# Expert stage of a one-core delta-rule and mixture-of-experts kernel: bulk transfers issued by ScalarE, copies of w1 left to the sync engine, sorted rows stored tile by tile

## What is computed

```python
# attention, per batch and head, over t
y[t] = q[t] @ state
state = state + beta[t] * outer(k_n[t], v[t] - k_n[t] @ state)
# experts: E = 8, F = 1024
e_idx = argmax(x @ w_gate + modality_bias[modality_id]);  gate_w = its softmax probability
out[mask_e] = gate_w * (relu(x[mask_e] @ w1[e]) @ w2[e])
# second layer: F2 = 768
h = maximum(maximum(x @ m2_w1, x @ m2_w2), x @ m2_w3);  result = h @ m2_out
```

## Time and profile before

| | us |
|---|---|
| median of 3 runs | 1092.8 (1092.8 to 1100.61) |
| the profiled execution | 1095.86 |
| its span | 1094.1 |
| mean granted clock of TensorE | 0.964 |
| TensorE busy in the span | 918.4 |
| ScalarE busy in the span | 480.7 |

### The profile page before, as it was taken

One profiled execution on the slowest core, in us unless ns is written; L12 is line 12 of the kernel. 1 busy time (PEld: TensorE's weight loads), 2 busy tenths in 40 slices (PEclk: granted clock), 3 DMA queues, 4 the chain that ended last, 5 costly groups with the idle time before them and its releaser, 6 DMA issues.

```text
span 1094.1 us, 29171 instructions
## 1 busy us (share of the span) xinstructions
PE 918.4 (84%) x10418; PEld 679.9 (62%) x10418; DVE 623.9 (57%) x1484; ACT 480.7 (44%) x1076; POOL 308.5 (28%) x810
## 2 busy tenths in 40 slices
PE   3258989888798888238998998997799999999998
PEld 3147878777797778226776776765554454545444
DVE  5337778767777767624884865943763324243322
ACT  3124656556465545624853736633542323323221
POOL 4646456767857553520000000001430000000000
PEclk9999889989989999659999999998999999999999
DMA  6366665655434441079639669479840000000000
GB/s 154 73 167 175 165 156 118 146 102 113 101 83 94 91 99 31 16 254 356 221 146 316 252 235 329 187 275 325 274 146 8 22 29 1 29 0 29 7 22 29
DMA packets 223333, 147.07 MB, mean 134 GB/s; under 512 B 162240, under 2 KB 200128, under 8 KB 223200
## 3 DMA queue, kind: packets, MB, share of 16 engines
q1 hardware_dynamic: 170208, 126.42, 37.2%
q10 hardware_dynamic: 49920, 9.44, 4.6%
q0 software_dynamic: 3072, 9.44, 2.7%
HBM read 69.63 MB, written 26.87 MB: 88 GB/s over the span
## 4 chain that ended last, share of the span: by engine, by line
PE 47%; POOL 15%; SPq 13%; issue 9%; DMA 8%; DVE 4%; ACT 2%; another core or an unknown queue 1%; DVEq 0%; POOLq 0%; ACTq 0%
PE psum L1617 19%; PE psum L1636 6%; PE psum L1566 5%; PE psum L1553 5%; POOL arena L637 4%; POOL arena L634 3%; SPq L554 3%; DMA arena<-arena 2%; SPq L529 2%; SPq L510 2%; DMA arena<-blocks 2%; SPq L558 2%; DMA arena<-in_moe_w_dram 1%; POOL arena L665 1%; PE psum L1470 1%
## 5 line engine op out<-in xcount | busy, mean ns | idle before, releaser
L1617 PE MATMUL psum<-arena 128*128 128x512 f16 x972 | 212.4, 379 | 0.3 <-issue 0.3
L1553 PE MATMUL psum<-arena 128*128 128x128 f16 x2232 | 148.8, 222 | 23.7 <-DMA arena<-arena 18.2
L1617 PEld LDWEIGHTS psum<-arena 128*128 128x128 f16 x972 | 95.0, 98 | 112.4 <-issue 0.7
L1553 PEld LDWEIGHTS psum<-arena 128*128 128x128 f16 x2232 | 135.8, 99 | 41.4 <-DMA arena<-arena 20.6
L1566 PE MATMUL psum<-arena 128*128 x744 | 144.1, 330 | 20.2 <-DVE arena L1211 9.1
L804 POOL DMA_INDIRECT arena<-y_sorted,arena x24 | 23.6, 982 | 319.2 <-DMA y_sorted<-arena 288.1
L1314 DVE SCALAR_TENSOR_TENSOR arena<-psum,arena 128x512 f32<-128x512 f32 x36 | 27.0, 751 | 146.5 <-PE psum L1617 146.5
L1566 PEld LDWEIGHTS psum<-arena 128*128 128x128 f16 x744 | 71.4, 97 | 59.6 <-issue 33.6
L971 ACT ACTIVATE arena<-psum 128x256 f16<-128x256 f32 x124 | 46.9, 378 | 95.8 <-PE psum L1553 90.0
L1211 DVE SCALAR_TENSOR_TENSOR arena<-psum,arena 128x256 f16<-128x256 f32 x124 | 52.1, 420 | 59.5 <-ACT arena L971 57.3
L1140 DVE SCALAR_TENSOR_TENSOR arena<-arena 128x384 f16<-128x384 f32 x128 | 73.1, 613 | 13.6 <-ACT arena L830 8.3
(11 more groups left out here) (198 smaller groups left out, 1807.4 us busy)
## 6 DMA issues: line engine op xcount, KB each, us to landing
arena<-arena SPq DMA_DIRECT2D x124, 384.0 KB
arena<-in_moe_w_dram SPq DMA_DIRECT2D x73, 384.0 KB, 4.8
arena<-inverses SPq DMA_DIRECT2D x24, 512.0 KB, 5.8
x_sorted<-arena SPq DMA_DIRECT2D x7, 768.0 KB, 6.0
arena<-in_k_dram SPq DMA_DIRECT2D x24, 192.0 KB, 3.7
arena<-in_v_dram ACTq DMA_DIRECT2D x24, 192.0 KB, 3.7
arena<-in_q_dram ACTq DMA_DIRECT2D x24, 192.0 KB, 4.5
out_dram<-arena SPq DMA_DIRECT2D x24, 192.0 KB, 1.9
```

The costliest lines, as they stand in the source:

```text
L1553: last = nc.tensor.matmul(psum[:, n % 2, fc * P:fc * P + P], w1[:, at:at + P], xT16[:, s, y, kc * P:kc * P + P], start=(i == 0), stop=(i = ...
L1617: last = nc.tensor.matmul(psum[:, 2 + 3 * (f % 2) + m, :], up_weight(w, m, kc, f), x16[:, par, kc, x, :], start=(i == 0), stop=(i == len(t ...
```

## The change

The loads of the experts' and the second layer's weights, the last three loads of sorted rows and the stores to y_sorted move from the sync engine to ScalarE, inside its loop over tiles, behind the ReLU (and, in pass 0, the turned rows) and ahead of square sums and splits: weight i at tile i + 1, store of tile s - 2 at tile s. Each store now covers one tile, with a count per part. The sync engine's loop holds only copies of w1. Square sums, total and splits of the second layer's weights come one tile later than before; those of the experts' weights (`weighed_in`, `split_in`) stay.

```diff
         LG = DM
         CUM = 2 * P
         SX = [0, 1, 3, 6, 11, 18, 24, NSLOT]
+        FIRST = 4
         block = ctx.enter_context(nc.Block())
-        AHEAD = 3
         HALVES = (slice(0, PC // 2), slice(PC // 2, PC))
         def weighed_in(s):
...
         def m2_weighed_in(s):
-            return [s - 3] if 3 <= s < NM + 3 else []
+            return [s - 4] if 4 <= s < NM + 4 else []
         def m2_split_in(s):
-            return [s - 17] if 17 <= s < NM + 17 else []
-        M2_SUMMED, M2_SCALED = 15, 16
+            return [s - 18] if 18 <= s < NM + 18 else []
+        def part_of(s):
+            return sum(1 for z in SY[1:-1] if s >= z)
+        M2_SUMMED, M2_SCALED = 16, 17
         ROWS_SUMMED, ROWS_SCALED, TURNED = (24, 25), 26, 27
         SPLIT = NT - 4
...
         def columns_after(f, last):
             return [] if last else {1: [0, 1], 3: [2]}.get(f, [])
+        def expert_weights(queue, qq, i):
+            e, f0 = i // 2, qq * FQ
+            if i % 2 == 0:
+                queue.dma_start(raw(qq, i).rearrange("p (c f) -> p c f", c=KC),
+                                w1[e, :, f0:f0 + FQ].rearrange("(c p) f -> p c f", p=P)).then_inc(w_in[i // 4], 16)
+            else:
+                queue.dma_start(raw(qq, i).rearrange("p (c n) -> p c n", c=FC),
+                                w2[e, f0:f0 + FQ, :].rearrange("(c p) n -> p c n", p=P)).then_inc(w_in[i // 4], 16)
+        def load_columns(queue, i):
+            a, z = SX[i], SX[i + 1]
+            queue.dma_start(acc[:, a:z, :], x_sorted[a * P:z * P, :].rearrange("(s p) d -> p s d", p=P)).then_inc(xs_in[i], 16)
         def groups_in_order(e, group):
...
             sp.dma_start(cst16[:, :], c16).then_inc(cst_in, 16)
             sp.dma_start(cst32[:, :], c32).then_inc(cst_in, 16)
             sp.dma_start(braw[0:B * H, :], beta.rearrange("b h s -> (b h) s")).then_inc(beta_in, 16)
-            def expert_weights(qq, i):
...
             def step(what, t):
                 if what == "k":
...
                                  inverses[pair % 2, :, t % 2].rearrange("p h x c -> p (h x c)")).then_inc(inv_in[t % 4], 16)
                 if what == "w":
                     if 4 <= t < 4 + 2 * E:
-                        expert_weights(0, t - 4)
+                        expert_weights(sp, 0, t - 4)
                     if 6 <= t < 14:
                         a, z = NSLOT * (t - 6) // 8, NSLOT * (t - 5) // 8
                         sp.dma_start(x_sorted[a * P:z * P, :].rearrange("(s p) d -> p s d", p=P),
                                      zrow.unsqueeze(1).to_broadcast([P, z - a, DM])).then_inc(zero_in, 16)
-            def load_columns(i):
-                a, z = SX[i], SX[i + 1]
-                sp.dma_start(acc[:, a:z, :], x_sorted[a * P:z * P, :].rearrange("(s p) d -> p s d", p=P)).then_inc(xs_in[i], 16)
             def copy_w1(n):
...
             sp.wait_ge(scat_in, 16 * NT)
             sp.wait_ge(s_ok, NT)
-            for i in range(4):
-                load_columns(i)
+            for i in range(FIRST):
+                load_columns(sp, i)
             sp.wait_ge(eid_ok, 1)
             sp.wait_ge(gate_ok, 3)
-            for n in range(AHEAD):
+            for n in range(NQ * NSLOT):
                 copy_w1(n)
-            def m2_weights(i):
...
-            def store_sorted(i):
-                a, z = SY[i], SY[i + 1]
-                sp.wait_ge(acc_ok, NSLOT * (NQ - 1) + z)
-                sp.dma_start(y_sorted[a * P:z * P, :].rearrange("(s p) d -> p s d", p=P), acc[:, a:z, :]).then_inc(ysort_in[i], 16)
-            for n in range(NQ * NSLOT):
-                qq, s = n // NSLOT, n % NSLOT
-                if n + 4 < len(SX) - 1:
-                    load_columns(n + 4)
-                if s < NP and qq < NQ - 1:
-                    if s == 0 and qq > 0:
-                        sp.wait_ge(ym_mm, NSLOT * qq)
-                    expert_weights(qq + 1, s)
-                if s < NM and qq == NQ - 1:
-                    if s == 0:
-                        sp.wait_ge(ym_mm, NSLOT * (NQ - 1))
-                    m2_weights(s)
-                if qq == NQ - 1 and s - 1 in SY[1:]:
-                    store_sorted(SY.index(s - 1) - 1)
-                if n + AHEAD < NQ * NSLOT:
-                    copy_w1(n + AHEAD)
-            store_sorted(NC - 1)
             with sp.Fori(0, NC) as c:
                 for b in range(B):
...
                 c = t // B
                 if t % B == 0:
                     pool.wait_ge(h_mm, NSLOT * (NQ - 1) + B * (c + 1))
-                    pool.wait_ge(ysort_in[c], 16)
+                    pool.wait_ge(ysort_in[c], 16 * (SY[c + 1] - SY[c]))
                 nc.gpsimd.indirect_dma_start(x2[:, t, :], None, y_sorted[0:SY[c + 1] * P, :],
                                              bass.IndirectOffsetOnAxis(ap=pos[:, t:t + 1], axis=0)).then_inc(gath_in[min(c, 2)], 16)
...
                 need(act, o_mm, c * B)
                 nc.scalar.activation(h16[:, f, 0], h2[:, f % 2, :], ACT.Copy).then_inc(hhi_ok, 1)
+            def m2_weights(i):
+                if i < 3 * KC:
+                    act.dma_start(m2_raw(i), (m2_w1, m2_w2, m2_w3)[i // KC][i % KC * P:(i % KC + 1) * P, :]).then_inc(w_in[i // 3], 16)
+                else:
+                    f = 2 * (i - 3 * KC)
+                    act.dma_start(m2_raw(i).rearrange("p (c n) -> p c n", c=2),
+                                 m2_out[f * P:(f + 2) * P, :].rearrange("(c p) n -> p c n", p=P)).then_inc(w_in[i // 3], 16)
+            def store_sorted(s):
+                act.wait_ge(acc_ok, NSLOT * (NQ - 1) + s + 1)
+                act.dma_start(y_sorted[s * P:s * P + P, :], acc[:, s, :]).then_inc(ysort_in[part_of(s)], 16)
+            act.wait_ge(scat_in, 16 * NT)
+            for i in range(FIRST, len(SX) - 1):
+                load_columns(act, i)
             columns(0)
             columns(1)
             for qq in range(NQ):
...
                     nc.scalar.activation(hT[:, n % 2, 0, :], psum[:, n % 2, 0:FQ], ACT.Relu).then_inc(hh_ok, 1)
                     if qq == 0 and s + 2 < NSLOT:
                         columns(s + 2)
+                    if s == 1 and qq > 0:
+                        act.wait_ge(ym_mm, NSLOT * qq)
+                    if qq < NQ - 1 and 1 <= s <= NP:
+                        expert_weights(act, qq + 1, s - 1)
+                    if qq == NQ - 1 and 1 <= s <= NM:
+                        m2_weights(s - 1)
+                    if qq == NQ - 1 and s >= 2:
+                        store_sorted(s - 2)
                     if qq < NQ - 1:
                         for i in weighed_in(s):
                             weigh(qq + 1, i)
...
                                 square_row(0, 0, B // 2 * ROWS_SUMMED.index(s) + b)
                         if TURNED < s <= TURNED + KC:
                             x_high(0, 0, s - TURNED - 1)
+            for s in (NSLOT - 2, NSLOT - 1):
+                store_sorted(s)
             def group(c, par, last):
                 for f in range(F2C):
```

More of the change, by code:

```diff
@@ L473, in _ @@
             sp.dma_start(braw[0:B * H, :], beta.rearrange("b h s -> (b h) s")).then_inc(beta_in, 16)
-            def expert_weights(qq, i):
-                e, f0 = i // 2, qq * FQ
-                if i % 2 == 0:
-                    sp.dma_start(raw(qq, i).rearrange("p (c f) -> p c f", c=KC),
-                                 w1[e, :, f0:f0 + FQ].rearrange("(c p) f -> p c f", p=P)).then_inc(w_in[i // 4], 16)
-                else:
-                    sp.dma_start(raw(qq, i).rearrange("p (c n) -> p c n", c=FC),
-                                 w2[e, f0:f0 + FQ, :].rearrange("(c p) n -> p c n", p=P)).then_inc(w_in[i // 4], 16)
             def step(what, t):
@@ L563, in _ @@
             sp.wait_ge(s_ok, NT)
-            for i in range(4):
-                load_columns(i)
+            for i in range(FIRST):
+                load_columns(sp, i)
             sp.wait_ge(eid_ok, 1)
             sp.wait_ge(gate_ok, 3)
-            for n in range(AHEAD):
+            for n in range(NQ * NSLOT):
                 copy_w1(n)
-            def m2_weights(i):
-                if i < 3 * KC:
-                    sp.dma_start(m2_raw(i), (m2_w1, m2_w2, m2_w3)[i // KC][i % KC * P:(i % KC + 1) * P, :]).then_inc(w_in[i // 3], 16)
-                else:
-                    f = 2 * (i - 3 * KC)
-                    sp.dma_start(m2_raw(i).rearrange("p (c n) -> p c n", c=2),
-                                 m2_out[f * P:(f + 2) * P, :].rearrange("(c p) n -> p c n", p=P)).then_inc(w_in[i // 3], 16)
-            def store_sorted(i):
-                a, z = SY[i], SY[i + 1]
-                sp.wait_ge(acc_ok, NSLOT * (NQ - 1) + z)
-                sp.dma_start(y_sorted[a * P:z * P, :].rearrange("(s p) d -> p s d", p=P), acc[:, a:z, :]).then_inc(ysort_in[i], 16)
-            for n in range(NQ * NSLOT):
-                qq, s = n // NSLOT, n % NSLOT
-                if n + 4 < len(SX) - 1:
-                    load_columns(n + 4)
```

(13 more changed lines are left out.)

## The result

The changed kernel takes 1144.55 us in the median (1137.13 to 1152.45, 4 runs), the kernel before 1095.15 in the runs beside it: a ratio of 1.0445, 95% interval 1.0358 to 1.0531. Slower was forecast, at 1112 and at most 1135. The sum behind that was +19.5 us; the loss is 49 us, outside the range. The profiled execution took 1141.96 us, 46.1 more than the one of before.

What follows compares the result with a forecast made beforehand. It took the sync engine's queue of copies and loads to bound the expert stage's loading tiles. Passes 1 to 3 +10, +6.8, +6.3, last pass -8.6, clock +5 gave +19.5 us: 1112 us, range 1080 to 1135.

Steps and rivals of the forecast that it cites:

- the last pass: Last pass of the expert stage: weight loads and tile-by-tile stores on ScalarE, -8.6 us, ends -18 and 0.
- part 4: TensorE's clock falls in half of the 12 waits, 0.8 us each: +5 us, ends 0 and +17.
- part 2: Passes 1 to 3: ScalarE waits for loads only just issued, +10, +6.8 and +6.3 us.
- the landing of 4.4 us: Passes 1 to 3: time from issue of an awaited weight load until its data are in, 4.4 us.
- 5.2 us for the three tiles behind a wait: Passes 1 to 3: after a wait, one tile at ScalarE's 1.75 us, two at TensorE's 1.98, less TensorE's lead: 5.2.
- The tiles behind them stay as they are: Passes 2 and 3: tiles after tile 17 keep their time, 0 us.
- Part 1: Sync engine without the loads: a loading tile's bound falls from about 2.5 to 1.98 us, if DMA keeps up.
- The start: Start of pass 1: sorted rows requested at once share DMA engines with the first copy, +4 us, ends 0 and +8.
- C: Rival, slower: landing 5.6 us (+14) and the clock falls mostly (+8), 1134 us; chance 0.12.
- A: Rival, faster: loads land in 3.1 us on ScalarE's queue, -12 us, 1081 us; chance 0.2.
- B: Rival, no difference: landing near 3.7 us, no clock fall, about 1096 us; chance 0.2.
- D: Rival: copies wait for DMA bandwidth, loading tiles stay at 2.5 us; sum changes by 3 at most; no separate chance.

Runs made afterwards that it cites:

- The short loads: Changed kernel with the expert weight loads of passes 2 to 4 cut to 128 and 192 KB, the rest not loaded: ratio 1.0215.
- The one-tile experiment: Changed kernel with only the square sums of the experts' weights one tile later: ratio 1.0021.
- the mended change: Changed kernel with the experts' square sums two tiles later and totals one tile later, splits kept: ratio 1.008.
- the sync engine's version: Kernel before with experts' square sums two tiles and totals one tile later, all transfers left on the sync engine: ratio 0.9985.

## Why the prediction was wrong

**What held.** The direction, and the main cause: ScalarE's in-order wait for load 4g + 3, 12 times in the first three passes, one right behind each issue, with the next ReLU behind it. The signs named for it came: 12 waits, long times from one ReLU to the next behind tiles 4, 8, 12 and 16 (5.6 to 7.8 us, where 5 to 6.5 were named), the clock at 0.50 behind a wait. Their size was off: waits of 3 to 4 us and about 40 in sum were named, and 4.7 and 56.2 came. The 40 did not fit the prediction's own sum either, which holds 12 waits of 4.3 us, 52. Undoing the distance removed the loss, and creating it elsewhere brought it back. The last stage did not change (the time after the last ReLU, +0.9).

**Where the sum missed.** The trace lost 46.1 us for 19.5, so 26.6 are to be explained. By differences of the ReLU rows, against the prediction's own terms: the times over the twelve waits +7.7; the tiles behind the waits +15.9 (10.7 in the groups of three, 5.2 behind the fourth wait of each pass), less the 5 that part 4 had put aside for the clock; the last pass +7.5; the rest and rounding +0.5. So three steps failed, all of them sizes, and the wait itself is not the largest.

**The first step that failed: the landing of 4.4 us in part 2**, and with it "while TensorE stands no new copies come, so I go a little under". It was taken from the median of all loads, and the median was right even afterwards: 4.2 us for ScalarE's loads on the page. But the load that decides is the last of four, issued when three before it and the copies are still moving. In pass 2 the first four landed after 3.9, 5.3, 5.9 and 6.9 us, each later than the one before. By the prediction ScalarE would have idled 0.28 + 4.4 - 0.38 = 4.3 us; it was 5.3 in the mean of the eight waits of passes 2 and 3 (42.0 us), and 3.6 in pass 1 (14.2), where tiles are longer and ask for less per us. The 0.28 was too long, which hid a part: the issue starts 0.01 us behind the ReLU's start (592.89, 592.90), so the awaited load landed after 5.6 us in the mean of these eight and 4.0 in pass 1. The short loads show that most of this is bytes and not a fixed time. In those tiles a load and a copy, 768 KB per 1.98 us, ask for 397 GB/s; the DMA engines gave 361 and 390 in the stretches from 592 to 596 us. Before, the sync engine's loop of 2.5 us asked for about 315 GB/s, which is near the 325 that the earlier trace rows show.

For pass 2 the sum is off by 8.7 us. The ReLU pairs over the four waits were 7.8, 6.5, 6.1 and 7.4, with 5.5, 5.5, 6.3 and 6.3 forecast: 4.2 of it. In pass 3 this step is worth 3.7, in pass 1 nothing.

**The second step, and the largest: 5.2 us for the three tiles behind a wait, nothing for those behind the fourth, and the clock of part 4.** They took 7.6 and 6.9 us after the waits at tiles 4 and 8, with 5.2 forecast, and 7.8 after tile 12, with 7.4: 4.5 us, the other half. The first such wait left TensorE idle for 3.17 us, not 2.4, and the next 24 matmuls took 4.23 us for 2.32. Over the kernel TensorE is busy 14.7 us more, where +5 was put, with an upper end of 17. The idle time was 3.1 us in the mean of the twelve, not 2.4, and the clock fell behind nine of them, not six; so there were 1.6 us of added busy time for each fall, where part 4 had put a loss of 0.8. "The tiles behind them stay as they are" had no reason behind it: behind the fourth wait, gaps of 3.6 to 4.7 us stood at tile 19, and the tiles from 17 on took, over the three passes, 98.6 us for 93.4. With the waits taken out and the splits kept they took 94.2. The one-tile experiment shows the other side, where at 2 us of wait both the delay and the added busy time are gone.

**The third step: the last pass**, -8.6 forecast, -1.1 in the two traces. The gap of the big store went as said (tile 15: 7.7 to 1.4 us), but gaps of 3.9 to 5.1 us stood at tiles 16, 19, 23, 27 and 30. With one and the same code for this pass it took 83.7, 76.9, 76.9, 87.7, 77.9 and 85.1 us in six profiled kernels; so the term can't be read from one trace. The runs with the stores alone put it at -3 us of the kernel (0.9971), and with later sums at nothing (1.0002). What makes these late gaps is open; the trace names "remote" for the one at tile 16.

**Part 1** was right as to the sync engine and wrong as to its worth. Its 2.5 us loop was the path, and a ceiling of the DMA engines lay just behind it, as the 0.95 share of the earlier trace rows said; 39 us had been reckoned for the 17 tiles by bytes, but 43 to 45 came. The rule of the Trainium skill cited there, that a second issuer saves only issue time, is borne out: 281 to 295 GB/s came from two queues and 305 to 310 from one. The mended change against the sync engine's version shows that here even this issue time buys nothing. The start was +6.7 us, forecast +4 with an end of +8; that the table shows +3.8 beside +4 is luck, since the attention stage ended earlier in that trace.

**The rivals.** C gave 1134, the nearest. Its landing of 5.6 is what the awaited loads of passes 2 and 3 took, and its clock term, +13 in all, is near the 14.7 us more of busy TensorE. What it lacked is what the forecast lacked too, the tiles behind the fourth wait and the last pass. Its remark that the issue itself would hold ScalarE was wrong: no issue of such a load took more than 0.40 us there. A and B fell with the landing. D has something to it, as the chain of the mended change shows: with the waits gone, the copies are late by the DMA engines and the loading tiles stay at 2.5 us. The Trainium skill's fixed time plus bytes ("DMA: Bandwidth & Descriptors", "Anatomy of one DMA"), named beside A with an estimate of 2.9 us, is stated for GpSimd's DMAs; here no load of 384 KB that ScalarE issued for the experts landed under 3.0 us, and the twelve that were awaited took 3.4 to 7.0, nearly twice 2.9 in the mean of passes 2 and 3.

## What to carry to other kernels

Before a load is moved to another engine, write down for each wait the tile in which its last load goes out: here one tile of distance was worth 4%, and with the waits eased all the rest of the change cost 0.2 to 1.3%. Price such a wait with the landing of the last load of its group while the others are under way, not with the median, and set against it what the bound engine still has ahead. Past that point add the lower clock behind the idle time, here 14.7 us of busy time for twelve waits, and the tiles in which the engines catch up, which cost more here than the error in the wait did. Where a path is issue-bound and the DMA engines stand at 0.95, relieving the issuer moves the bound and not the time.

## What the runs showed of the hardware

The issue of a 384 KB load took 0.39 us on ScalarE (line 404, 387 ns in the median) and 0.59 on the sync engine, for the same transfer. The issue did not hold ScalarE: the longest of line 404 was 0.40 us, where the sync engine's reached 2.05, and it began 0.01 us behind the start of a ReLU (592.89, 592.90) and ran beside it. A wait of 2.0 us in the mean, 11 times, cost next to nothing, one of 4.7, 12 times, over 40 us.

Of two idle times of TensorE of nearly one length the clock need not take the same course: behind 1.95 us at 618 us the next output product took 1.15 us and the granted clock of 617 to 619 us was 1.00; behind 1.94 us at 706 us the product took 1.15 us as well, but the next hidden product took 1.90, and the granted clock from 708 to 710 us was 0.50.
